# Attention, router and expert kernel on one core: first weights loaded later, x stored in thirds, the last x scaled on ScalarE, and TensorE products into a spare bank

## What is computed

```python
kv = einsum('bhsd,bhse->bhde', k, v)            # batch 8, heads 8, seq 576, dim 64
out = einsum('bhsd,bhde->bhse', q, kv)
x = out / sqrt(mean(out * out) + 1e-6) * g_norm # 4608 rows of 512
# first mixture: each row goes to its best of 8 experts
e = argmax(x @ w_gate);  y = gate * sigmoid * (relu(x @ w1[e]) @ w2[e])
# second mixture: 4608 (row, expert) pairs taken in order of score, 576 rows to each expert
out[mask] = relu(y[mask] @ w21[e]) @ w22[e]
```

## Time and profile before

| | us |
|---|---|
| median of 3 runs | 1413.93 |
| lowest, highest | 1410.87, 1417.98 |
| the profiled execution | 1408.05 |
| its span | 1406.3 |

### The profile page before, as it was taken

One profiled execution on the slowest core, in us unless ns is written; L12 is line 12 of the kernel. 1 busy time (PEld: TensorE's weight loads), 2 busy tenths in 40 slices (PEclk: granted clock), 3 DMA queues, 4 the chain that ended last, 5 costly groups with the idle time before them and its releaser, 6 DMA issues.

```text
span 1406.3 us, 21870 instructions
## 1 busy us (share of the span) xinstructions
PE 1247.8 (89%) x7584; PEld 1001.0 (71%) x7584; DVE 980.6 (70%) x2363; ACT 447.0 (32%) x804; POOL 383.6 (27%) x324
## 2 busy tenths in 40 slices
PE   6888619898999999999999218999999999999996
PEld 5787517787888888888887116677777777777884
DVE  2676793777667677776678687888888888886621
ACT  2665532222222222222222022333232323233421
POOL 2244436747523361743000001111111111111110
PEclk8999859999999999999999558999999999999998
DMA  9999328695415151551110032332323231414100
GB/s 212 253 279 293 134 56 307 223 372 171 150 46 160 51 158 38 166 161 51 39 39 23 8 127 67 119 96 93 111 78 126 70 135 53 149 40 150 46 30 19
DMA packets 70119, 172.22 MB, mean 122 GB/s; under 512 B 11624, under 2 KB 30136, under 8 KB 69376
## 3 DMA queue, kind: packets, MB, share of 16 engines
q1 hardware_dynamic: 46576, 108.61, 25.5%
q0 software_dynamic: 11344, 40.02, 8.8%
q10 hardware_dynamic: 12096, 22.19, 4.8%
HBM read 129.42 MB, written 41.37 MB: 121 GB/s over the span
## 4 chain that ended last, share of the span: by engine, by line
PE 73%; DMA 8%; DVE 8%; POOL 6%; issue 2%; ACT 2%; SPq 0%; POOLq 0%; ACTq 0%; DVEq 0%
PE bank L759 53%; PE bank L831 4%; PE bank L777 4%; POOL w_lo L594 3%; DMA x_rows<-xrow 2%; DMA xst<-x_rows,tok_i 2%; PE bank L887 2%; PE bank L824 2%; PE o_ps L727 1%; PE kv_ps L685 1%; DMA x_sorted<-xst 1%; DMA q_sb<-in_q 1%; POOL w_hi L592 1%; DMA w_sb<-in_moe_w 1%; PE bank L814 1%
## 5 line engine op out<-in xcount | busy, mean ns | idle before, releaser
L1386 DVE SCALAR_TENSOR_TENSOR bank<-bank,factor,wg2b 128x512 f32<-128x512 f32 x336 | 254.5, 758 | 10.4
L1352 DVE TENSOR_TENSOR hT_lo<-bank,hT_hi 128x512 fp32r<-128x512 f32 x150 | 96.4, 684 | 171.0 <-ACT hT_hi L1093 170.0
L1050 ACT ACTIVATE h<-bank 128x512 f32<-128x512 f32 x166 | 99.4, 599 | 311.2 <-PE bank L759 307.1
L759 PE MATMUL bank<-w_hi,xT_hi 128*128 (+1 forms) x600 | 175.7, 415 | 8.2 <-POOL w_lo L594 4.3
L649 POOL DMA_INDIRECT xg<-y_rows,gat_i x40 | 39.5, 988 | 493.2 <-DVE sca_i L1509 380.0
L759 PE MATMUL bank<-w_lo,xT_hi 128*128 (+1 forms) x600 | 173.7, 405 | 0.0
L759 PE MATMUL bank<-w_hi,xT_lo 128*128 (+1 forms) x600 | 167.3, 400 | 0.0
L759 PE MATMUL bank<-w_hi,hT_hi 128*128 (+1 forms) x600 | 159.9, 408 | 6.0 <-DVE score L1389 4.5
L759 PE MATMUL bank<-w_lo,hT_hi 128*128 (+1 forms) x600 | 158.8, 401 | 0.0
L759 PE MATMUL bank<-w_hi,hT_lo 128*128 (+1 forms) x600 | 155.5, 398 | 0.0
L594 POOL TENSOR_TENSOR w_lo<-w_sb,w_hi 128x1024 fp32r<-128x1024 f32 x56 | 134.4, 2399 | 4.5
(11 more groups left out here) (257 smaller groups left out, 1790.5 us busy)
## 6 DMA issues: line engine op xcount, KB each, us to landing
w_sb<-in_moe_w SPq DMA_DIRECT2D x112, 512.0 KB, 5.5
y_rows<-y ACTq DMA_DIRECT2D x43, 256.0 KB, 2.9
x_sorted<-xst SPq DMA_DIRECT2D x41, 260.0 KB, 5.3
xg<-x_sorted ACTq DMA_DIRECT2D x41, 260.0 KB, 2.7
x_rows<-xrow POOLq DMA_DIRECT2D x16, 585.0 KB, 7.8
k_sb<-in_k SPq DMA_DIRECT2D x16, 576.0 KB, 19.6
v_sb<-in_v SPq DMA_DIRECT2D x16, 576.0 KB, 18.7
q_sb<-in_q SPq DMA_DIRECT2D x8, 1152.0 KB, 20.5
```

What stands on the lines that cost most here:

```text
L759: mm = pe.matmul(ps, a[:, i % chunks, :], b[:, i % chunks, cols], start=(i == 0), stop=(i == 3 * chunks - 1))
L1050: act.activation(h[:, half * HALF:(half + 1) * HALF], h_ps[half][:, :], ACT.Copy if short else ACT.Relu).then_inc(s_h, 1)
L1352: dve.tensor_tensor(hT_lo[:, half * 4:(half + 1) * 4, :].rearrange("p a b -> p (a b)"), th_ps[half][:, :], hT_hi[:, half * 4:(half + 1) * ...
L1386: ch.link(dve.scalar_tensor_tensor(out=prod_ps[:, :], in0=y1_ps[t % 2][:, :], scalar=factor[:, t:t + 1], in1=wg2b[:, e, :], op0=ALU.mult, ...
```

## The change

It has four parts.

1. SyncE waits, ahead of the first expert's weights, until the third part of x of the first six batches is stored.
2. `x_rows` is stored in three parts of two tiles. VectorE waits for them at c = 0, 2 and 4.
3. The last batch's x is multiplied on ScalarE, in 48 instructions of 96x64 (8 to a tile), half of them ahead of `ex` and half behind `ez`. `first_high` moves behind the one-hots, and the second router's copy behind the first of those. GpSimd only stores.
4. TensorE gets `kept_running(times)`: that many products of ones, 128x512 in float16, into the bank `th_ps[1]`, whose result nobody reads. They stand ahead of the second and third group of one-hots (5 and 4), behind the last group (20), and behind the steps of the first and the opening of the second search (2 or 7 by turns, and 1, 3, 16 and 12 at single places).

```diff
+            sp.wait_ge(s_xst[X_PARTS - 1], 16 * (B - 2))
             for n in range(2):
                 load_half(0, n, s_wl)
...
             for b in range(B):
-                pool.wait_ge(s_rin, b + 1)
+                if b < B - 1:
+                    pool.wait_ge(s_rin, b + 1)
                 for c in range(CT):
...
+                    elif c % part == part - 1:
+                        pool.wait_ge(s_xa, c + 1)
+                    if c % part == part - 1:
+                        n = c // part
...
+            def kept_running(times):
+                for _ in range(times):
+                    pe.matmul(th_ps[1][:, :], ones_h[:, :], ones_h[:, :].unsqueeze(1).to_broadcast([P, 4, P]),
+                              start=True, stop=True)
...
+                        kept_running((0, 5, 4)[n])
                         pe.wait_ge(s_ohb, n + 1)
...
+            kept_running(20)
             pe.wait_ge(s_par, 1)
...
+            IN_WAIT = {SUMS: 1, TOTALS: 3, TIES: 16}
...
             for n in range(STEPS):
                 search(0, n)
+                kept_running(IN_WAIT.get(n, 2 if n % 2 == 0 else 7))
             for n in range(LISTED + 1):
                 search_and_list(1, n)
+                kept_running(12 if n == LISTED else 2 if n % 2 == 0 else 7)
...
-            first_high()
+            def last_x(slices):
+                for c in slices:
+                    for n in range(H):
+                        cols = slice(n * D, (n + 1) * D)
+                        scaled_x = act.activation(xrow[(B - 1) % 2][:, c, cols], xrow[(B - 1) % 2][:, c, cols], ACT.Copy,
+                                                  scale=rin[(B - 1) % 2][:, c * H + n:c * H + n + 1])
+                    scaled_x.then_inc(s_xa, 1)
+
+            act.wait_ge(s_rin, B)
+            last_x(range(CT // 2))
             act.wait_ge(s_sh, B)
             act.activation(ex[:, :, :], sh[:, :, :], ACT.Exp).then_inc(s_ex, 1)
             act.wait_ge(s_zs, 1)
             act.activation(ez[:, :], zs[:, :], ACT.Exp, scale=-1.0).then_inc(s_ez, 1)
+            last_x(range(CT // 2, CT))
...
-                    if c % 3 == 0:
-                        wait_pos(dve, s_xst[c // 3], (e - 1) * 16)
+                    if c % (CT // X_PARTS) == 0:
+                        wait_pos(dve, s_xst[c * X_PARTS // CT], (e - 1) * 16)
```

More of the change, by code:

```diff
@@ L76, in build @@
     NT2 = E * T2
+    X_PARTS = 3
     MIDDLE = S * B // 2 - PT * CT // 2
@@ L241, in build @@
         s_xn = sem("x_normed")
+        s_xa = sem("last_x_normed")
         s_fst = sem("factor_stored")
@@ L247, in build @@
         s_fa = sem("factor_ready")
-        s_xst = [sem(f"x_stored{c}") for c in range(2)]
+        s_xst = [sem(f"x_stored{c}") for c in range(X_PARTS)]
         s_dve = sem("dve_chain")
@@ L507, in _ @@
             sp.wait_ge(s_fa, 1)
-            for n in range(2):
+            for n in range(X_PARTS):
                 sp.wait_ge(s_xst[n], 16 * B)
@@ L595, in split_piece @@
                                    ALU.subtract).then_inc(s_split, 1)
-            third = CT // 2
+            part = CT // X_PARTS
             for b in range(B):
-                pool.wait_ge(s_rin, b + 1)
+                if b < B - 1:
+                    pool.wait_ge(s_rin, b + 1)
                 for c in range(CT):
[L601 to L606, removed]
+                    if b < B - 1:
+                        xv = xrow[b % 2][:, c, 0:DM].rearrange("p (h d) -> p h d", d=D)
+                        pool.tensor_tensor(xv, xv, rin[b % 2][:, c * H:(c + 1) * H].unsqueeze(2).to_broadcast([PT, H, D]),
+                                           ALU.mult).then_inc(s_xn, 1)
+                        pool.wait_ge(s_xn, b * CT + c + 1)
+                    elif c % part == part - 1:
+                        pool.wait_ge(s_xa, c + 1)
+                    if c % part == part - 1:
+                        n = c // part
                         wait_pos(pool, s_xst[n], b * 16)
-                        pool.dma_start(x_rows[b * S:(b + 1) * S, :].rearrange("(p c) n -> p c n", c=CT)[:, n * third:(n + 1) * third, :],
-                                       xrow[b % 2][:, n * third:(n + 1) * third, :]).then_inc(s_xst[n], 16)
-            for n in range(2):
+                        pool.dma_start(x_rows[b * S:(b + 1) * S, :].rearrange("(p c) n -> p c n", c=CT)[:, n * part:(n + 1) * part, :],
+                                       xrow[b % 2][:, n * part:(n + 1) * part, :]).then_inc(s_xst[n], 16)
+            for n in range(X_PARTS):
                 pool.wait_ge(s_xst[n], 16 * B)
@@ L1042, in _ @@
                 act.activation(ra1[:, gs, :, 1], oha1[:, gs, :], ACT.Copy, scale=row1[:, 0:1]).then_inc(s_rar, 1)
-            act.wait_ge(s_wgt, 1)
-            act.activation(h[0:E, 0:DM], bank[3][0:E, :], ACT.Copy).then_inc(s_wgc, 1)
+                if n == 0:
+                    act.wait_ge(s_wgt, 1)
+                    act.activation(h[0:E, 0:DM], bank[3][0:E, :], ACT.Copy).then_inc(s_wgc, 1)
+            first_high()
             def relu(n, short=False):
```

## The result

| | before | after |
|---|---|---|
| median of 4 runs, us | 1414.24 | 1395.99 |
| lowest, highest | 1410.87, 1417.98 | 1394.53, 1397.62 |
| the profiled execution, us | 1408.05 | 1397.62 |
| its span | 1406.3 | 1395.9 |

The ratio of the medians is 0.9871, with a 95% interval from 0.9842 to 0.9899. The forecast of 1394 and its range hold. But the two profiled executions lie only 10.4 us apart, where the sum said 19.5. So the trace is read stretch by stretch first.

What follows compares the result with a forecast made beforehand. Attention bound by DMA, then VectorE's chain to the token list, GpSimd's gathers to 348.80 us, then TensorE, with searches at half clock. -13 - 1.8 - 0.4 - 4.3 = -19.5 from the median 1413.93 gives 1394 us, range 1384 to 1404.

Steps and rivals of the forecast that it cites:

- the offset of 5.9 us: Whole kernel: the profiled execution, 1408.05 us, lies 5.9 us under the median of the runs, 1413.93.
- Attention, -13: Attention: late weights and stores in thirds remove VectorE's waits for stores; -13 us, between -6 and -19.
- without the 7.75 us wait the distance is 15.6 us: Attention: first tiles of batches 5 and 6, at 118.12 and 141.47, would lie 15.6 us apart without that wait.
- The term of 4 us for the loads: Attention: about two more stores moved by then delay the last v's landing by 4 us, from 130.6 to 134.6.
- only the weights matter: Rival, attention: thirds land no sooner, short waits all but stay; attention gives 8, total 1399.4 us; chance 0.17.
- Routing, -2.2: Routing: last x on ScalarE, -1.8 us (0 to -3.5), and products of ones among the one-hots, -0.4 (0 to -0.5).
- The 20 products, 0: Behind the last one-hots: 4.6 us of products fit a wait of 5.16; TensorE waits for GpSimd anyway, gain 0.
- The searches, -4.3: Opening searches and phases' start: products of ones keep TensorE's clock up; -4.3 us, between -6 and +11.
- the cold seven: Searches: seven products ahead of a count, 3.6 us cold in a 1.89 us gap, delay the first by about 0.5.
- the 0.6 for the second search: Second search's opening: warm counts gain about 0.6 us; elsewhere other work of VectorE's hides it.
- the 2.0 of the phases' start: Phases' start: beginning warm, 24 products take 5.60 us instead of 8.01, of which 2.0 is taken as gain.
- three signs of error: TensorE waits over 5 us for v at batch 7; factor stored after the token list; counts start late behind products.

Runs made afterwards that it cites:

- six_parts: The changed kernel with x stored in six parts of one tile, each waited for at its own tile; 1394.90 us, ratio 0.9899.
- stores_and_weights: The kernel before with only the stores in thirds and the late first weights; 1399.86 us, ratio 0.9919.
- fuller: The changed kernel with more products of ones in the opening searches, where TensorE was cold; 1394.94 us, ratio 0.9892.

## Why the prediction was right or wrong

**The number.** 1394 against 1395.99, inside the range. But it came out of a sum of 19.5 us on a median of three runs, 1413.93, and both were high. On the three chips of the experiments the kernel before had medians of 1411.15, 1407.54 and 1411.64 us, over 11 to 22 runs each, nearer to the profiled 1408.05. The changed kernel, run again, was 1398.83: 12.8 us less than before, against 18.2 in the first comparison. The ledger says 10.4 for one pair of executions. In its last row 1.5 of the 2.0 us are a fall of the clock at the very end that varies between traces; the 1.1 us above it came again when the kernel was run again and belong to the change. That makes 12, and I take 12 to 13 us for what the change is worth. That the forecast lies within 2 us of the measured time is luck. It had stated the offset of 5.9 us and kept it only in the range.

**Attention, -13: the step that failed** is "without the 7.75 us wait the distance is 15.6 us". A wait was subtracted from a distance, as if the engine had nothing else to wait for. The engines need 17.07 us (six_parts). With it the gain is 127.69 - 117.16 = 10.5 at most, and the change had 9.4 of it in one trace and 10.3 in the other. Most of that lies in the long wait, 23.35 - 17.07 = 6.3, and 2.9 in the first one. The term of 4 us for the loads was void: with all store waits gone no engine waited for a load from 40 us on. The weights were issued at 151, not 142, and hidden as forecast.

**The thirds.** The first of a batch landed in 8.2 to 8.8 us against 8.9 for a half (8.7 to 9.3 over all batches); what was estimated by bytes (a third less data, 1.7 us) did not come. The Trainium skill's rule (DMA: Bandwidth & Descriptors, Queues, rings and completion order), that engines take turns between queues packet by packet, agrees with this row; no run looks at the turns themselves. The short waits shrank from 9.1 to 3.3 us all the same, by the earlier issue of about 1 us a batch and since a part of each had never counted. So the rival "only the weights matter" (attention 8) was nearer in its size than the forecast's 13. Its reason was half right: the thirds landed no sooner, but the short waits did not stay. They shrank, and it brought only 1.0 us.

**Routing, -2.2:** 2.4 measured. `ex` is ready 7.9 us after the last `rin`, forecast 8.2 (0.243 us for each of 24, forecast 0.25), and VectorE waits 1.74 for it, forecast "0 to 2". Its parts were not seen rightly: 0.5 to 0.85 of the 2.4 came from the thirds, and ScalarE's part brought 1.17 of its 1.8.

**The 20 products, 0:** right; but the wait at expert 2 did not grow to 6 us. It was 2.46, none in stores_and_weights, and between 1.7 and 8.4 in the other kernels. A single value of such a wait says little.

**The searches, -4.3: mis-sized.** Measured -0.8 in the two openings, +1.1 at the phases' start, and -0.25 for all products by the medians on one chip. A warm round's gain was right (0.29 for 0.3). Wrong were the cold seven (0.70, twice, for 0.5 once), the 0.6 for the second search (+0.4 instead), and the 2.0 of the phases' start. Such a start is worth 1.7 to 2.0, but the change doesn't keep it warm, and behind the later wait the clock falls where it had not before.

**What would show it:** waits for stores 3.8, not near 0; the token list at 193.8, not 190; L1284 and L1289 (L1255 and L1260 before) at 0.20 for the last batch, but L1284 at 1.07 for the first six, where it had been so for two of eight; clock 1.0 from the third count on, not the second; counts at 0.48 there. Of the three signs of error the third appeared: two counts came late behind products.

## What to carry to other kernels

A wait can be subtracted from a period only down to what the engines need without it. The busiest engine's time in one period (here 16.0 us of TensorE) is the floor to look up first, and 15.6 was below it. A wait that goes may leave nothing behind but another wait: the last 3.8 us of waits for stores were worth nothing here. Two cures for one wait don't add up, so each wants to be priced as if the other were there. Here the products that were to hold the clock paid only where every wait of the stretch was filled (fuller) and the first fill wasn't itself in the way; and a gain of 2 us in one stretch was undone by the clock in the next.

## What was not expected of the hardware

Beside the same loads, from 60 us on, a store of 585 KB took 8.4 us from issue to landing (median of 7 in the kernel before), one of 390 KB 7.4 (12 in the changed kernel) and one of 195 KB 6.8 (25 in six_parts): a third of the bytes takes four fifths of the time. The first store of a batch, the one that VectorE comes to first, landed in 8.7 to 9.3, 8.2 to 8.8 and 7.8 to 8.5 us. The granted clock fell at a wait of 2.04 us in some executions and held in others of nearly the same program: the transposes right behind it were cold (1.97 us for eight) in eight of fourteen traces and warm (1.16) in six. The count between took 0.72 us in five of the eight, and 0.48 to 0.59 in three, where the clock fell while it ran or right behind it. TensorE's last products (L790 in the changed kernel) ran partly at 1.2 GHz behind a wait of 2.41 us in eleven traces, and at 2.4 GHz throughout in three: from the last transposes of gathered rows to the end it is 36.0 or 34.5 us, 1.5 us that no part of the change decides. And one VectorE instruction of 0.20 us took 1.08 in one of two traces of the same program, where it met a multiplication of GpSimd's.
